# A reordered first batch, two output products moved into the last batch's stage, and a shorter routing chain

## The reference

```python
def _attn_ref(q, k, v):                     # (4, 8, 576, 64)
    # causal local attention: heads 0 to 3 see the last 32 keys,
    # heads 4 to 7 every 4th of the last 128
...
def _moe_ref(x, w_gate, wq, wk, wv, wo):    # 4 experts of causal attention, top 2
...
def _moe2_ref(x, w_gate, w_local, w1, w2):  # 8 experts, one for each token
    ...
            fresh_e = int(np.argmax(logits[b, s]))
            if s == 0 or local_gate[b, s] < 0.5:
                e = fresh_e
            else:
                e = prev_e if prev_e >= 0 else fresh_e
            ...
            h = np.maximum(x[b, s] @ w1[e], 0.0)
            out[b, s] = p[e] * (h @ w2[e])
```

## Time and profile before

| | us |
|---|---|
| median of 3 executions | 703.81 (702.8 to 704.96) |
| the profiled execution | 705.35 |
| its span | 703.60 |
| TensorE busy | 692.2 (98%) |
| VectorE busy | 302.9 (43%) |
| ScalarE busy | 286.4 (41%) |
| GpSimd busy | 97.3 (14%) |

### The profile page before, as it was taken

The page is one execution under the profiler, slowest core; times in us unless marked ns, Lnnn a source line. Parts: engine busy times, 40 slices in busy tenths (PEclk is TensorE's granted clock), DMA queues, the critical chain, the costliest instruction groups (busy, mean ns, idle before and its releaser), DMA issues.

```text
span 703.6 us, 15555 instructions
## 1 busy us (share of the span) xinstructions
PE 692.2 (98%) x5225; PEld 514.9 (73%) x5226; DVE 302.9 (43%) x916; ACT 286.4 (41%) x865; POOL 97.3 (14%) x138
## 2 busy tenths in 40 slices
PE   8999999999999999999999999999999999999997
PEld 7888777787677777776667777776777777677774
DVE  5744897168852888326666211121111211122111
ACT  4853777258672596515510222223222232222320
POOL 4310011000000001000022211122111211122113
PEclk9999999999999999999999999999999999999999
DMA  7793028231461214200144143701421770001101
GB/s 171 166 228 95 20 67 217 80 69 27 108 195 45 60 27 108 103 7 2 46 177 140 45 159 134 262 30 59 177 107 34 270 280 29 30 30 45 38 30 38
DMA packets 86787, 69.59 MB, mean 99 GB/s; under 512 B 69166, under 2 KB 69694, under 8 KB 86736
## 3 DMA queue, kind: packets, MB, share of 16 engines
q1 hardware_dynamic: 79136, 44.73, 22.9%
q0 software_dynamic: 7600, 24.19, 10.2%
HBM read 118.12 MB, written 11.27 MB: 184 GB/s over the span
## 4 chain that ended last, share of the span: by engine, by line
PE 94%; SPq 2%; DVE 1%; DMA 1%; issue 1%; POOL 0%; ACT 0%; DVEq 0%; POOLq 0%
PE bank L1328 22%; PE bank L1339 21%; PE bank L818 9%; PE bank L814 5%; PE bank L912 5%; PE bank L739 4%; PE bank L897 4%; PE bank L868 4%; PE bank L779 4%; PE bank L839 3%; PE bank L752 2%; PE bank L710 2%; PE bank L717 2%; PE bank L1311 1%; PE bank L844 1%; PE bank L930 1%
## 5 line engine op out<-in xcount | busy, mean ns | idle before, releaser
L1328 PEld LDWEIGHTS bank<-pt,stage_b 128*128 128x128 f32 x1344 | 155.0, 192 | 10.0 <-issue 10.0
L1339 PE MATMUL bank<-w_all,raw_all 128*128 x352 | 158.2, 592 | 0.0
L1328 PE MATMUL bank<-pt,stage_b 128*128 128x128 f32 x1344 | 156.9, 275 | 0.0
L1806 ACT ACTIVATE raw_all<-bank 128x512 f32<-128x512 f32 x44 | 26.3, 597 | 214.6 <-PE bank L1328 214.6
L1339 PEld LDWEIGHTS bank<-w_all,raw_all 128*128 128x128 f32 x352 | 63.6, 190 | 63.6 <-issue 63.6
L2405 DVE TENSOR_SCALAR raw_all<-bank,p_slot 128x512 f32 x21 | 15.8, 751 | 209.1 <-PE bank L1339 209.1
L631 POOL DMA_INDIRECT out_dram<-raw_all,idx_out x25 | 37.6, 1505 | 246.9 <-DVE raw_all L2405 230.0
L818 PE MATMUL bank<-stage_b,w_all 128*128 128x288 f32 x256 | 68.2, 412 | 0.5 <-issue 0.5
L1519 ACT ACTIVATE pr<-sm,negmax_a 96x80 f32<-96x80 f32 (+1 forms) x168 | 59.6, 359 | 2.8 <-DVE negmax_a L1858 2.8
L818 PEld LDWEIGHTS bank<-stage_b,w_all 128*128 128x128 f32 x256 | 46.6, 190 | 14.5 <-issue 3.7
L1508 ACT COPY w_sb<-bank 128x256 f32<-128x256 f32 (+5 forms) x93 | 38.0, 419 | 30.0 <-PE bank L868 27.7
(11 more groups left out here) (231 smaller groups left out, 896.7 us busy)
## 6 DMA issues: line engine op xcount, KB each, us to landing
w_sb<-in_moe_w_dram SPq DMA_DIRECT2D x19, 2048.0 KB
w_all<-in_moe_w_dram SPq DMA_DIRECT2D x19, 2048.0 KB
w_sb<-in_moe_w_dram POOLq DMA_DIRECT2D x12, 512.0 KB, 4.9
w_all<-in_moe_w_dram POOLq DMA_DIRECT2D x12, 512.0 KB, 5.2
mixture_rows<-y_sb SPq DMA_DIRECT2D x16, 256.0 KB, 2.0
raw_all<-in_q_dram SPq DMA_DIRECT2D x28, 144.0 KB
raw_all<-in_k_dram SPq DMA_DIRECT2D x28, 144.0 KB
v_dil<-in_v_dram SPq DMA_DIRECT2D x42, 80.0 KB, 3.6
```

Of the source, the lines that this page charges most:

```text
L1328: last = pe.matmul(ps[half][:, f * P:(f + 1) * P], w1_sb[:, 0, c * F + at:c * F + at + P] if buf is None else w1_fix[:, c, at:at + P], xT[ ...
L1339: last = pe.matmul(ps[5], hidT[:, half * HALF + n * P:half * HALF + (n + 1) * P], w2_sb[:, bass.ds(buf, 1), half, n * D:(n + 1) * D].rearr ...
```

## The change

**First batch.** The lists of the three engines are reordered. `pe_probs` of groups 1 to 6 stand one step earlier or so, `pe_router_turn` stands behind the probabilities of group 4 and no longer behind those of group 2, and the head transposes 11 to 14 lie elsewhere. VectorE's `dve_norm` and ScalarE's `move_probs` move in the same way. The numbers of constants change: 2 become 1 and 2 in the early part; 3 become 2, and 2 become 1, in the late part.

On TensorE in the first batch, from the value products of group 0 to the router transposes (L941 before, L949 now), the list was

The core of the diff; of the first batch's lists one piece stands:

```diff
@@ -189,6 +189,8 @@
+        e9 = [sb(f"e9_{i}", [P, EF + 1]) for i in range(2)]
+        per_expert, slots_to = e9[0][:, 1:], e9[1][:, 1:]
...
@@ -606,6 +610,10 @@
             pool.sem_inc(rows_stored, 1)
+            pool.wait_ge(rank_ready, 1)
+            pool.wait_ge(reach_ready, 1)
+            pool.tensor_tensor(token_hot, reach, c_token[:, :].unsqueeze(2).broadcast_to([P, LT, SLOTS + 1]), ALU.mult
+                               ).then_inc(token_hot_ready, 1)
             pool.wait_ge(row_ready, 1)
...
-            pe_router_turn(pe, None)
             pe_values(pe, a, 2)
             pe_probs(pe, a, 3)
...
             pe_probs(pe, a, 4)
+            pe_router_turn(pe, None)
...
@@ -1150,7 +1159,8 @@
-            pe_out(pe, m, a, 3, 16, 4)
+            if a < B - 1:
+                pe_out(pe, m, a, 3, 16, 4)
...
@@ -1160,12 +1170,12 @@
-            pe_out(pe, m, a, 4, 16, 4)
+            if a < B - 1:
+                pe_out(pe, m, a, 4, 16, 4)
...
         def pe_last(pe, m):
 
-            x_free(pe, m, None, 16, 0)
...
-            turn_over(pe, X, 8)
+            pe_out(pe, m - 1, None, 3, 16)
...
             pe_project(pe, m, 12)
+            pe_out(pe, m - 1, None, 4, 16)
...
-            pe_out(pe, m, None, 0, 16)
...
-            turn_over(pe, PA, 3)
+            pe_out(pe, m, None, 0, 16)
...
@@ -1716,10 +1726,12 @@
             act_exp2(act, m, 2, 0)
+            move_y(act_copy, act, m - 1, 3)
             act_exp2(act, m, 2, 1)
...
             act_exp2(act, m, 3, 0)
+            move_y(act_copy, act, m - 1, 4)
             act_exp2(act, m, 3, 1)
...
@@ -2252,24 +2264,24 @@
-            red(e8[0][:, :], fillc[:, :, :], ALU.add)
-            step(v_.tensor_tensor_scan(e8[1][:, :], ones[:, 0:EF], e8[0][:, :], 0.0, ALU.mult, ALU.add))
-            tt(e8[2][:, :], e8[1][:, :], e8[0][:, :], ALU.subtract)
...
+            red(e9[0][:, 1:], fillc[:, :, :], ALU.add)
+            step(v_.tensor_tensor_scan(e9[1][:, :], ones[:, 0:EF + 1], e9[0][:, :], 0.0, ALU.mult, ALU.add))
...
             v_.tensor_tensor(reach, along(r1[0][:, :], SLOTS + 1), over(c_slot[:, :], LT), ALU.is_ge).then_inc(reach_ready, 1)
             dve.wait_ge(reach_ready, 1)
-            v_.tensor_tensor(token_hot, reach, along(c_token[:, :], SLOTS + 1), ALU.mult).then_inc(token_hot_ready, 1)
 
             step(v_.tensor_copy(rank_i[0][:, :], r1[0][:, :]))
             step(v_.tensor_single_scalar(rank_i[1][:, :], rank_i[0][:, :], P - 1, ALU.bitwise_and))
             step(v_.tensor_copy(r1[1][:, :], rank_i[1][:, :]))
+            dve.sem_inc(rank_ready, 1)
...
-            step(v_.tensor_copy(tok[:, :], ps[2][:, 0:SLOTS + 1]))
-            tt(tok[:, 0:SLOTS], tok[:, 0:SLOTS], tok[:, 1:SLOTS + 1], ALU.subtract)
-            ts(idx_f[:, 0, 0:SLOTS], tok[:, 0:SLOTS], -1.0, ALU.add, 0.0, ALU.max)
-            v_.tensor_copy(idx[:, 0, :], idx_f[:, 0, :]).then_inc(row_ready, 1)
+            step(v_.tensor_copy(tok[:, 0:SLOTS], ps[2][:, 1:SLOTS + 1]))
+            tt(tok[:, 0:SLOTS], ps[2][:, 0:SLOTS], tok[:, 0:SLOTS], ALU.subtract)
+            v_.tensor_scalar(idx[:, 0, 0:SLOTS], tok[:, 0:SLOTS], -1.0, 0.0, ALU.add, ALU.max).then_inc(row_ready, 1)
```

115 lines of the change are left out of this document (60 added, 55 removed).

## The result

The changed kernel takes 699.42 us (median of 5 executions, 698.71 to 700.74), the kernel before 703.81. The ratio of the two is 0.9926, with a 95% interval of 0.9909 to 0.9944: between 3.9 and 6.4 us faster. Forecast were 697.4 and a range of 695.0 to 701.2; the forecast saving of 6.4 us is the upper end of that interval. The two profiled executions differ by more than the medians: spans 703.60 and 697.7, 5.9 us.

The account below looks back on a forecast made before the run. TensorE, busy 692.2 of 703.6 us, was taken as the bound, with overrunning constants and one long load wait on its chain. Gains 2.0 + 1.3 + 3.1 = 6.4 off the 703.8 median gave 697.4, range 695.0 to 701.2.

Parts of the forecast that it names:

- (b): Routing: GpSimd starts token_hot only after VectorE's three comparisons; 1.75 us of the gain goes, 699.1; chance 0.15.
- (e): Routing: with constants gone TensorE stands longer and its clock falls to 1.2 GHz, costing 2 us, 699.4; chance 0.04.
- (c): First batch and moved products give little because VectorE and ScalarE set the pace; 699.9; chance 0.13, with or without (b).
- First batch, 2.0: First batch: reordered lists remove the router-load wait and fewer late constants overrun; gain 2.0 us, bounds 0.5 to 2.0.
- term of 1.48: First batch: TensorE's 1.48 us wait for the router load before the router transposes, taken as wholly gone.
- late constants: Late first batch: 3 constants become 2 and 2 become 1, at 0.26 us each, gaining 0.5.
- Border and last stage, 1.3: Two output products move into the last batch's stage: 2.0 us gained at the border, 0.7 given back; bounds 0.3 to 1.9.
- Routing, 3.1: Between last batch and first slot: earlier scan, fewer constants and operations, token_hot on GpSimd; first slot 3.1 us earlier.
- Step (2): Routing: 5 constants before the counts become 3, so counts wait for VectorE's second scan; 0.94 us earlier in all.
- Step (5): Routing: token_hot takes 1.2 us on GpSimd (VectorE needs 0.70), its time adding to the comparisons; cumulative gain 1.8.
- Rival (a): Routing: GpSimd and VectorE do not hinder each other; last products start about 1.0 us earlier, 696.4; chance 0.12.
- (d): Routing: token_hot on GpSimd takes many times a copy; at 8.8 us all 6.4 are gone, at 11, 706.0; chance 0.03.

Follow-up runs that it names:

- the two runs above: Changed kernel with GpSimd's token_hot waiting for reach alone: median 699.23, ratio 0.9932; changed kernel with that product executed twice on GpSimd: median 703.6, ratio 0.9981.

## Why the prediction was right, point by point

- **The total.** 699.42 lies in the range, but also within half a microsecond of what rivals (b), (e) and (c) give (699.1, 699.4, 699.9). The number alone does not tell them from the forecast; the landmarks and the experiments do.
- **First batch, 2.0.** The wait went, as said, and no wait for VectorE came in its place. The size was off: 1.73 in the two profiled executions, 1.7 over 13 when the offset of the first loads is taken out. The term of 1.48 was read from the execution with the longest wait; over five it is 1.30 on average. The late constants gave 0.60 where 0.5 was put, but the added constant of the early part, counted at nothing because VectorE would cover it, stands on the chain with 0.22.
- **The sum set against the median.** The prediction saw that the profiled execution took 1.54 us more than the median and let the 6.4 be taken from the median all the same. Its first projection started 0.4 later than the mean of five: 0.2 of that was the longer router wait, which the change takes away, and 0.2 the late first loads, which it does not. A term that varies from execution to execution is worth its mean, not its value in the profile at hand. The ratio gives 5.2 us, 1.2 short of the 6.4: 0.3 of that is the first batch (1.7 in place of 2.0) and 0.2 the first slot's transposes. The other 0.7 is less than its interval can tell. Falls of the clock may lie in it: in the run of the first batch alone, executions with a mean granted clock of 0.998 or more took 703.55 to 703.99, and those at 0.997 took 705.00 to 705.30.
- **Border and last stage, 1.3.** 1.24. The gain at the border is 2.0 as worked out, with a wait of 0.61 where 0.7 was put, and the last stage gives back 0.76 where 0.6 to 0.7 was put. ScalarE was in time. The cause of the wait was only half seen: a copy of ScalarE ends at the same time as the normalisation, so making VectorE faster there gives 0.05.
- **Routing, 3.1.** 3.15. By steps, counted from the output product: the scan 0.47 earlier (0.55), the counts 0.68 (0.94), the comparisons 1.37 (1.75), the row index 1.88 (2.0). Step (2) was too large by 0.2. The sum and the epsilon now stand between the two scans, and the transposes were ready (357.99) before they were done (358.13); that makes less than 0.1. The rest lies between the end of the second scan and the counts: 0.72, 0.99 in the kernel before, where the forecast leaves 0.61.
- **Step (5), GpSimd.** 1.06 where 1.2 was taken; the comparisons were stretched by 0.91. The Trainium skill's figure (GPSIMD Engine Reference, Performance versus the Vector engine) gave an estimate of 1.14, within 0.1 of it. On this product GpSimd is 1.06 / 0.70 = 1.5 times slower than VectorE, against the factor of nearly two that the Trainium skill has for 2048 columns. Rival (a) is out, since the two runs above show the engines taking turns, and so is (b).
- **What the sum hid.** Step (5) says in its own numbers that the move costs 1.2 and saves 0.70. The text passed over this, in a row of gains. The move to GpSimd is a loss of 0.4 us on the row index, of which next to nothing reached the first slot in the two profiles without it; the constants carry the routing (2.65 of 2.9).
- **Rival (e), the clock,** had 0.04 and a price of 2. The standing was worked out as 1.6 and is 1.65. In the execution first profiled the clock held; in the second it fell, for 0.67 us, and with 0.8 us more of standing it fell again. It is more likely and cheaper than it was put. **Rival (c)** and **(d)** did not happen.

## What to carry to other kernels

A constant product ahead of a wait costs its overrun, and it can be read from the chain of waits: if TensorE never waits behind it, it is too long; but cut it down to the wait and not to nothing, for without it the clock falls and the dense work behind pays. Before a wait in a profile is counted as a gain, see how it varies between executions, above all one for a load, and take off the median its mean, not its value in the profile at hand. And measure the gain from a landmark ahead of the change, so that an offset of the whole execution drops out. A product handed from VectorE to GpSimd is no gain by itself: here VectorE's next operations need SBUF in the same way, and the product was queued against its own successors.

## What the runs showed of the hardware

- The granted clock can fall without any wait of TensorE: in two of 14 profiles it fell to 0.50 at 352 to 353 us, behind products of 9 and 64 columns, for some 3.5 us, at a cost of 1.7 us. The other profiles ran the same products without a fall.
- At the same standing (1.65 us) it fell in one execution and held in three.
- A cast of 20 columns that takes 0.18 us took 0.98 while GpSimd read SBUF; GpSimd's product of 520 columns took 1.06 us when it came first and 1.94 when it came behind a comparison.
- The same gather of 128 rows landed 3.5 to 4.0 us after its issue in 13 profiles and 5.37 in one. Loads still under way ahead of it go with 3.95 and 4.00, but 3.9 and 5.37 came without them or with as few as at 3.59.
- From the head transposes near 15 us to the first projection eight executions took 30.36 or 30.37 us; what varied between executions was when the loads landed.
